# An early Exp-table load, a later second value block, and another step for the next expert's weight split, in a fused attention and mixture-of-experts kernel

## The chip, the core and the metric

The kernel runs on one core of a Trainium2 chip, as one launch. The metric is the device time of the launch in microseconds, as the median of several executions. The host only lays the inputs out.

## What is computed

Sizes: B = H = 8, S = 512, 32 state rows, D = 64; 4352 tokens of 512 channels come out of the attention.

```
scores = x @ state.T / 8 ; xread = softmax(scores) @ state          # every token reads the states
scores2 = state @ x.T / 8 ; sread = softmax(scores2) @ x            # every state reads the tokens
x1 = concat(xread, sread), laid out as [4352, 512]
h  = x1 @ w_in ; x2 = max(0.01*h, h) @ w_out                        # 512 -> 2048 -> 512
e  = argmax(x2 @ w_gate) ; weight = softmax(...)[e] * sigmoid(x2 @ w_output_gate)[e]
out = weight * (relu(x2 @ w1[e]) @ w2[e])                           # 8 experts, 512 -> 1024 -> 512
```

## The kernel before, in words

Every large product is three TensorE (PE) matmuls on numbers split in a high and a low fp32r part (product, L499 to L503: hi times lo, lo times hi, hi times hi). ScalarE (ACT) writes the high parts, VectorE (DVE) subtracts to get the low ones. An order written out by hand sets what each engine does; semaphores join them. There are two phases.

**Phase one** runs over nine blocks b (eight batches and the state rows), each in 16 steps f (layer, L739 on PE, L969 on ACT, L1339 on DVE). The attention's read is folded into the first product: make_v (L528) forms a value block v(b, k), which is the states times 512 columns of w_in; keep_v (ACT, L893) and v_rest (DVE, L1155) split it. Step f does up(b, f) (L618), then down(b, f-2) (L643) into four accumulator banks. Between the two, ACT scales by 0.01 (L927), DVE takes the maximum (L1176), ACT casts to gT_hi (L933), DVE subtracts for gT_lo (L1180). Small work of the neighbouring blocks is put beside these steps (beside_up, L662, and beside_down, L688). For block 0 that is flip_a2 at steps 3 and 4, read_states(0) (L544) at step 4 behind down(0, 2), turn_read(0) (L556) at step 5. The copies that these wait for or feed are DVE's keep_a2 (L1134), keep_read (L1140) and keep_sread (L1145). The eight w_out pieces are split by split_piece (L873, L1074) at the steps that PIECE_AT names.

Before the first step comes a head (L755 to L761): first_scores_T twice, make_v(0, 0), scores_T(0), make_v(0, 1) into acc[0:2]; down(0, 0) writes the same banks, and so waits for v_rest(0, 1) (L648). ACT's head is L1007 to L1015: two exp_rows, keep_v(0, 0), two a_hi, split_piece(0), keep_v(0, 1), two exp_T. DVE's head is L1419 to L1436; its last part is max_T twice, split_piece(0), v_rest(0, 1).

**Phase two** sorts tokens by expert. A step i takes 256 tokens of one expert (tiles = 2), or, as the last step of an expert, 128 (a half step, tiles = 1). Here there are 21 steps for five experts: steps 0 to 10 for the first and largest, 11 to 13, 14, 15 to 17 and 18 to 20; steps 10, 13, 14, 17 and 20 are half steps. Step 0 is written out (L825); steps 1 on are loops. In a step PE does the hidden product (L769, L788) and the output product (L810 to L823), which needs h_lo_done as it goes. DVE's expert_step (L1547) makes hT_lo(0) to hT_lo(4), then turn_quarters(i + 1) (L1329: it transposes the next step's rows xq and copies s_in, once both have landed), then the other three, rows_lo, and the splits. POOL's load_rows (L409) brings the next rows from DRAM: five DMAs on its queue, when s_taken says that the buffer is free.

The next expert's weights are split into w_hi, w_lo (split_expert, L960, L1309; eight pieces, the first four are w1) in the first looped step of an expert (i < first + 1), on ACT behind rows_hi(i + 1), on DVE six behind rows_lo(i + 1) and two at the end of the step. PE starts an expert once e_lo_done tells of its four w1 pieces (L802). SP loads the raw weights (load_planned, L362): w1 when the w1 pieces before are split, w2 when all eight are; the first time behind rows_in 160, the rows of steps 0 and 1. Counts and columns are read from the small tensor ctl, written by DVE (L1500 to L1509). POOL's loop over the experts (L465) reads three of them for each.

Of the kernel before, what the change touches and what calls it, by code (L numbers as in the profile page):

```python
# [26 lines left out]
PIECE_AT = {0: 1, 3: 2, 5: 3, 6: 4, 10: 5, 12: 6, 14: 7}  # L27
# [8 lines left out]
def build(nc, xT_in, x_in, stT_in, st_in, w_in, w_out, w_gates, w1, w2, consts, tri_in, slot_init, out):  # L36
# [7 lines left out]
    with ctx:  # L44
# [238 lines left out]
        CTL_POOL = 35  # L283

# [4 lines left out]
        def _(sp):  # L289
# [70 lines left out]
            sp.wait_ge(rows_in, 160)  # L360
# [22 lines left out]
        def _(pool):  # L383
# [81 lines left out]
            with pool.Fori(0, E) as v:  # L465
                first, end = load_ctl(pool, v + CTL_POOL, MAXP, 1), load_ctl(pool, v + CTL_POOL + 1, MAXP, 1)
                col0 = load_ctl(pool, v + 17, COLS)
                with pool.If(first < end):
                    with pool.Fori(first, end) as sent:
                        n = pool.snap(sent + 2)  # L470
                        col = nc.s_assert_within(pool.snap(col0 + (sent - first) * 2), 0, COLS - 2,
                                                 skip_runtime_bounds_check_because="an expert has room for all tokens")
                        pool.wait_ge(pairs_clear[1], 16 * clear_in(1, PAIRS))
                        pool.wait_ge(s_taken, n)
                        load_rows(col)
                        next_tokens(n)
                        pool.wait_ge(slots_in, 16)
                        pool.wait_ge(toks_shifted, n)
                        pool.tensor_copy(tok_next[:, :], slot_tok[:, bass.ds(col, 2)]).then_inc(toks_kept, 1)
                        scatter(n)  # L480
# [17 lines left out]
        def _(pe):  # L498
# [163 lines left out]
            def beside_up(b, f):  # L662
# [14 lines left out]
                elif f == 5 and r is None:  # L677
# [10 lines left out]
            def beside_down(b, f):  # L688
# [11 lines left out]
                elif f == 4 and r is None:  # L700
# [38 lines left out]
            def layer(b):  # L739

                for f in range(F1):
                    if b == 0 and f == 0:
                        first_up()
                    elif b < B:
                        up(b, f)
                    else:
                        up_states(f)
                    beside_up(b, f)
                    if f >= 2:
                        down(b, f - 2)  # L750
                    beside_down(b, f)
# [7 lines left out]
            pe.wait_ge(half_turned, 2)  # L759
            make_v(0, 1, to=acc[0:2])  # L760
# [111 lines left out]
        def _(act):  # L872
# [39 lines left out]
            def beside_g(b, f):  # L912
                a, r = b + 1 if b < B - 1 else None, b - 1 if b > 0 else None
                if r is not None and f in (1, 2, 4):
# [54 lines left out]
            def layer(b):  # L969
                a, r = b + 1 if b < B - 1 else None, b - 1 if b > 0 else None  # L970
                for f in range(F1):
                    g_step(b, f)
                    if b == 0 and f in PIECE_AT:
# [32 lines left out]

            exp_rows(0, 0)  # L1007
# [5 lines left out]
            keep_v(0, 1, of=acc[0:2])  # L1013
            exp_T(0, 0)
            exp_T(0, 1)  # L1015
# [15 lines left out]
            def expert_step(i, tiles, first, c1, c2, v, s):  # L1031
# [6 lines left out]
                if v + 1 < E:  # L1038
# [21 lines left out]
            c0, c1 = load_ctl(act, 0, MAXP), load_ctl(act, 1, MAXP)  # L1060
            for v in range(E):
                cf = load_ctl(act, v + CTL_FULL, MAXP)
                c2 = load_ctl(act, v + 2, MAXP) if v + 1 < E else c1
                with act.If(c0 < cf):
                    with act.Fori(c0, cf) as i:
                        expert_step(i, 2, c0, c1, c2, v, v % 2)
                with act.If(cf < c1):
                    expert_step(cf, 1, c0, c1, c2, v, v % 2)
                c0, c1 = c1, c2
# [3 lines left out]
        def _(dve):  # L1073
# [362 lines left out]
            v_rest(0, 1, of=acc[0:2])  # L1436
# [53 lines left out]
            def plan_steps():  # L1490
# [15 lines left out]
                dve.tensor_scalar(ctl[:, 26:27], end[:, 7:8], 2.0, None, ALU.add)  # L1506
                dve.tensor_scalar(ctl[:, 44:45], end[:, 7:8], 80.0, 80.0, ALU.mult, ALU.add)
# [39 lines left out]
            def expert_step(i, tiles, first, c1, c2, v, s):  # L1547
# [11 lines left out]
                if v + 1 < E:  # L1559
                    with dve.If(i < first + 1):  # L1560
                        with dve.If(c1 < c2):
                            split_expert(v + 1, 1 - s, range(6))
# [9 lines left out]
                if v + 1 < E:  # L1572
                    with dve.If(i < first + 1):
                        with dve.If(c1 < c2):
                            split_expert(v + 1, 1 - s, range(6, 8))

            c0, c1 = load_ctl(dve, 0, MAXP), load_ctl(dve, 1, MAXP)
            for v in range(E):
                cf = load_ctl(dve, v + CTL_FULL, MAXP)
                c2 = load_ctl(dve, v + 2, MAXP) if v + 1 < E else c1  # L1580
                with dve.If(c0 < cf):
                    with dve.Fori(c0, cf) as i:
                        expert_step(i, 2, c0, c1, c2, v, v % 2)
# [50 lines left out]
```

## Time and profile before

| | us |
|---|---|
| median of 3 runs | 1141.16 (1140.4 to 1143.56) |
| the profiled execution's own time | 1135.01 |
| its span | 1133.3 |
| PE busy in the span | 1106.1 |
| DVE, ACT, POOL busy | 623.1, 401.3, 207.4 |

The span is the profiled execution from its first to its last instruction. PE is busy in 98% of it. Its idle time is the place to look: a wait of PE with an engine named behind it lengthens the kernel by about its own length, since PE has no slack elsewhere.

### The profile page before, as it was taken

How to read it: one execution, taken by the hardware profiler on the slowest of the kernel's cores; microseconds unless marked ns; L12 is line 12 of the kernel's file. 1: busy time of each engine (PE TensorE's matmuls, PEld its weight loads, DVE VectorE, ACT ScalarE, POOL GpSimd, SP SyncE). 2: the span in 40 equal slices, each digit the busy share in tenths (PEclk: the TensorE clock that was granted, in tenths of full speed). 3: DMA queues.
4: the chain of work that ended last, by engine and by line, in shares of the span. 5: the costliest groups of instructions: out<-in, count | busy, mean ns of one | idle time of the engine just before them, and what ended most of it. 6: DMA issues, size and time to landing. Idle time of an engine off the chain costs nothing.

```text
span 1133.3 us, 18114 instructions
## 1 busy us (share of the span) xinstructions
PE 1106.1 (98%) x6514; PEld 895.9 (79%) x6515; DVE 623.1 (55%) x1364; ACT 401.3 (35%) x751; POOL 207.4 (18%) x298
## 2 busy tenths in 40 slices
PE   5999999999999999999999999999999999989997
PEld 2777777777777777777777889989998989878895
DVE  6584484674754854845744566673343336366342
ACT  3444334334434433443344355241121124244121
POOL 1000011020020020110110303532232232333222
PEclk9999999999999999999999999999999999999999
DMA  9398197394692890930130301691111122545111
GB/s 337 115 297 245 57 295 213 123 310 132 186 310 71 247 301 27 307 101 1 38 75 8 124 1 39 149 266 55 56 49 44 37 75 70 168 96 145 40 37 40
DMA packets 73007, 149.85 MB, mean 132 GB/s; under 512 B 11231, under 2 KB 12511, under 8 KB 72928
## 3 DMA queue, kind: packets, MB, share of 16 engines
q1 hardware_dynamic: 59696, 115.34, 35.3%
q0 software_dynamic: 13248, 33.71, 9.8%
q8 instruction: 36, 0.59, 0.2%
q14 instruction: 27, 0.22, 0.1%
HBM read 131.11 MB, written 92.01 MB: 197 GB/s over the span
## 4 chain that ended last, share of the span: by engine, by line
PE 87%; DVE 6%; DMA 3%; ACT 2%; issue 2%; POOLq 0%; POOL 0%; SPq 0%; DVEq 0%; ACTq 0%
PE bank L501 27%; PE bank L503 26%; PE bank L502 26%; PE bank L534 3%; PE bank L552 1%; DMA raw<-w_dram 1%; PE bank L568 1%; DMA s_in<-rows_dram 1%; DVE w_lo L1313 1%; PE bank L576 1%; PE bank L512 1%; ACT w_hi L967 1%; PE bank L541 1%; DVE g_buf L1176 1%; DMA XT<-xT_in_dram 1%
## 5 line engine op out<-in xcount | busy, mean ns | idle before, releaser
L501 PE MATMUL bank<-wout_lo,gT_hi 128*128 128x512 f32 x544 | 215.9, 397 | 0.0
L503 PE MATMUL bank<-wout_hi,gT_hi 128*128 128x512 f32 x544 | 212.3, 390 | 0.0
L502 PE MATMUL bank<-wout_hi,gT_lo 128*128 128x512 f32 x544 | 212.0, 390 | 0.0
L1176 DVE TENSOR_TENSOR g_buf<-g_buf,bank 128x512 f32<-128x512 f32 (+1 forms) x144 | 94.2, 654 | 107.5 <-ACT g_buf L927 107.4
L501 PE MATMUL bank<-xgT_lo,w_hi 128*128 128x256 f32 x512 | 144.8, 283 | 2.9 <-DVE w_lo L1313 2.6
L503 PE MATMUL bank<-xgT_hi,w_hi 128*128 128x256 f32 x512 | 143.8, 281 | 0.0
L502 PE MATMUL bank<-xgT_hi,w_lo 128*128 128x256 f32 x512 | 143.8, 281 | 0.0
L1180 DVE TENSOR_TENSOR gT_lo<-g_buf,gT_hi 128x512 fp32r<-128x512 f32 (+1 forms) x144 | 95.4, 662 | 72.9 <-ACT gT_hi L933 71.4
L927 ACT ACTIVATE g_buf<-bank 128x512 f32<-128x512 f32 (+1 forms) x144 | 82.5, 573 | 147.1 <-PE bank L503 145.6
L933 ACT CAST gT_hi<-g_buf 128x512 fp32r<-128x512 f32 (+1 forms) x144 | 85.9, 597 | 136.5 <-DVE g_buf L1176 136.5
L403 POOL DMA_INDIRECT rows_dram<-y_buf,row_i x34 | 35.0, 1031 | 542.0 <-DVE row_i L1270 534.4
L1022 ACT ACTIVATE hT_hi<-bank 128x256 fp32r<-128x256 f32 x128 | 49.2, 385 | 217.1 <-PE bank L503 217.1
L501 PEld LDWEIGHTS bank<-wout_lo,gT_hi 128*128 128x128 f32 x544 | 102.2, 188 | 26.4 <-DVE gT_lo L1180 5.4
L503 PEld LDWEIGHTS bank<-wout_hi,gT_hi 128*128 128x128 f32 x544 | 102.1, 188 | 22.5
L501 PE MATMUL bank<-w_lo,hT_hi 128*128 128x512 f32 x296 | 116.4, 393 | 2.2 <-DVE hT_lo L1441 1.5
L502 PEld LDWEIGHTS bank<-wout_hi,gT_lo 128*128 128x128 f32 x544 | 102.3, 188 | 20.2
L503 PE MATMUL bank<-w_hi,hT_hi 128*128 128x512 f32 x296 | 115.5, 390 | 0.0
L502 PE MATMUL bank<-w_hi,hT_lo 128*128 128x512 f32 x296 | 115.4, 390 | 0.0
L501 PE MATMUL bank<-aT_lo,v_hi 128*128 128x512 f32 x254 | 107.9, 425 | 2.1 <-DVE g_buf L1176 1.4
L501 PEld LDWEIGHTS bank<-xgT_lo,w_hi 128*128 128x128 f32 x512 | 96.4, 188 | 5.0 <-issue 3.8
L503 PE MATMUL bank<-aT_hi,v_hi 128*128 128x512 f32 x254 | 100.0, 394 | 0.0
L502 PE MATMUL bank<-aT_hi,v_lo 128*128 128x512 f32 x254 | 99.7, 393 | 0.0
(216 smaller groups left out, 1697.3 us busy)
## 6 DMA issues: line engine op xcount, KB each, us to landing
rows_dram<-x_in_dram SPq DMA_DIRECT2D x17, 4128.0 KB, 25.2
xq<-rows_dram POOLq DMA_DIRECT2D x88, 128.0 KB, 2.8
raw<-w_dram SPq DMA_DIRECT2D x20, 512.0 KB, 7.8
raw<-w_dram SPq DMA_DIRECT2D x10, 1024.0 KB, 11.1
X<-x_in_dram SPq DMA_DIRECT2D x8, 1024.0 KB, 12.4
XT<-xT_in_dram SPq DMA_DIRECT2D x7, 1024.0 KB, 5.6
win<-w_in_dram SPq DMA_DIRECT2D x4, 1024.0 KB, 11.9
y_buf<-w_out_dram POOLq DMA_DIRECT2D x6, 512.0 KB, 6.2
```

The costliest lines, as they stand in the source:

```text
L403: pool.indirect_dma_start(out=rows_dram, out_offset=bass.IndirectOffsetOnAxis(ap=row_i[:, t:t + 1], axis=0), in_=y_buf[:, t, :], in_offset ...
L501: pe.matmul(o, l_hi, r_lo, start=first, stop=False)
L502: pe.matmul(o, l_lo, r_hi, start=False, stop=False)
L503: return pe.matmul(o, l_hi, r_hi, start=False, stop=last)
L512: last = pe.matmul(aux[g][NS * c:NS * c + NS, :], stT[a % 2][rows, c, cols], XT[rows, c, :], start=True, stop=True)
L534: last = pe.matmul(to[g][NS * c:NS * c + NS, :], stT[b % 2][rows, c, cols], win[rows, c, VW * k:VW * k + VW], start=True, stop=True)
L541: last = pe.transpose(to[:, P * t:P * t + P], a2T[:, g, P * t:P * t + P], ident)
L927: act.mul(g_buf[:, n, 0:w], up_b[n][:, 0:w], 0.01).then_inc(scaled, 1)
L933: act.copy(gT_hi[f % 4][:, 0:w], g_buf[:, n, 0:w]).then_inc(g_hi_done, 1)
L1022: act.activation(hT_hi[:, f, :], h_b[f % 4][:, :PAIR], ACT.Relu).then_inc(h_hi_done, 1)
L1176: dve.tensor_tensor(g_buf[:, n, 0:w], g_buf[:, n, 0:w], up_b[n][:, 0:w], ALU.max).then_inc(g_ready, 1)
L1180: dve.tensor_tensor(gT_lo[f % 4][:, 0:w], g_buf[:, n, 0:w], gT_hi[f % 4][:, 0:w].bitcast(fp32), ALU.subtract).then_inc(g_lo_done, 1)
```

## The change

For block 0: an Exp on a small tensor is the first thing ACT does; make_v(0, 1) goes behind up(0, 1); keep_v(0, 1) and v_rest(0, 1) go behind the work on step 0; exp_T(0, 1) goes between the two ACT parts of step 0; split_piece(1) goes from step 0 to 1; read_states(0) and turn_read(0) go one step later, and so do keep_read and keep_sread. For the experts: the split of the second expert's weights goes to step 2 (the smallest of 2 and the first expert's last step), the first raw load waits for the rows of step 2 (rows_in 240), and where the step with the split is a half step, the first two pieces go between its parts. POOL's loop over the experts is written out eight times, and the first expert's start is a constant.

```diff
-PIECE_AT = {0: 1, 3: 2, 5: 3, 6: 4, 10: 5, 12: 6, 14: 7}
+PIECE_AT = {1: 1, 3: 2, 5: 3, 6: 4, 10: 5, 12: 6, 14: 7}
...
+        CTL_SPLIT = 45
...
-            sp.wait_ge(rows_in, 160)
+            sp.wait_ge(rows_in, 240)
...
-            with pool.Fori(0, E) as v:
-                first, end = load_ctl(pool, v + CTL_POOL, MAXP, 1), load_ctl(pool, v + CTL_POOL + 1, MAXP, 1)
-                col0 = load_ctl(pool, v + 17, COLS)
...
+            first, col0 = 1, pool.snap(first_col + 4)
+            for v in range(E):
+                end = load_ctl(pool, v + CTL_POOL + 1, MAXP, 1)
+                if v > 0:
+                    col0 = load_ctl(pool, v + 17, COLS)
                 with pool.If(first < end):
                     with pool.Fori(first, end) as sent:
+                        send_step(sent, first, col0)
+                first = end
...
-                elif f == 5 and r is None:
+                elif f == 6 and r is None:
                     turn_read(0)
...
-                elif f == 4 and r is None:
+                elif f == 5 and r is None:
                     read_states(0)
...
+                    if b == 0 and f == 1:
+                        pe.wait_ge(half_turned, 2)
+                        make_v(0, 1, to=acc[0:2])
                     beside_up(b, f)
...
             scores_T(0)
-            pe.wait_ge(half_turned, 2)
-            make_v(0, 1, to=acc[0:2])
...
+                if b == 0 and f == 0:
+                    exp_T(0, 1)
...
                     g_step(b, f)
+                    if b == 0 and f == 0:
+                        keep_v(0, 1, of=acc[0:2])
...
+            act.wait_ge(rank_read, 1)
+            act.activation(edif[:, 0, :], before[:, 0, :], ACT.Exp)
             exp_rows(0, 0)
...
             split_piece(0)
-            keep_v(0, 1, of=acc[0:2])
             exp_T(0, 0)
-            exp_T(0, 1)
...
-            def hidden_rows(i):
+            def hidden_rows(i, piece):
                 for j in range(2):
                     act.wait_ge(h_ready, F2 * i + 4 * j + 1)
                     act.activation(h_rows[:, 4 * P * j:4 * P * j + 4 * P], h_b[j][:, :], ACT.Relu).then_inc(h_hi_done, 1)
+                    if j == 1:
+                        piece(1)
                     act.wait_ge(h_ready, F2 * i + 4 * j + 4)
                     act.copy(hT_hi[:, 4 * j:4 * j + 4, 0:P], h_b[2 + j][:, :].rearrange("p (f t) -> p f t", f=4)).then_inc(h_hi_done, 3)
+                    if j == 0:
+                        piece(0)
...
-                    with act.If(i < first + 1):
-                        with act.If(c1 < c2):
-                            split_expert(v + 1, 1 - s)
+                def pieces(which):
+                    if v + 1 < E:
+                        with act.If(i == split_at):
+                            with act.If(c1 < c2):
+                                split_expert(v + 1, 1 - s, which)
                 if tiles == 2:
                     hidden_T(i)
+                    rows_hi(i + 1)
+                    pieces(range(8))
                 else:
-                    hidden_rows(i)
-                rows_hi(i + 1)
+                    hidden_rows(i, lambda n: pieces((n,)))
+                    rows_hi(i + 1)
+                    pieces(range(2, 8))
...
-            c0, c1 = load_ctl(act, 0, MAXP), load_ctl(act, 1, MAXP)
+            c0, c1, split_at = 1, load_ctl(act, 1, MAXP), load_ctl(act, CTL_SPLIT, 2, 1)
...
-                c0, c1 = c1, c2
+                c0, c1, split_at = c1, c2, c1
...
-                    if b == 0 and f == 1:
+                    if b == 0 and f == 0:
+                        v_rest(0, 1, of=acc[0:2])
+                    elif b == 0 and f == 1:
                         norm_T(0, 0)
                         norm_T(0, 1)
...
                         keep_a2(0, 1, aux[1])
+                    elif b == 0 and f == 5:
                         keep_read(0)
-                    elif b == 0 and f == 5:
+                    elif b == 0 and f == 6:
                         keep_sread(0)
...
             split_piece(0)
-            v_rest(0, 1, of=acc[0:2])
...
+                dve.tensor_scalar(ctl[:, CTL_SPLIT:CTL_SPLIT + 1], end[:, 0:1], -1.0, 2.0, ALU.add, ALU.min)
...
                     h_lo_turned(i, 0)
+                    pieces(range(2))
                     h_lo_turned(i, 1)
                 rows_lo(i + 1)
...
+                pieces(range(2 if tiles == 1 else 0, 6))
...
+                pieces(range(6, 8))
```

## Rows read from the trace of the kernel before

**Rows 1.** The page, part 1: busy time of each engine.
```profile
PE 1106.1 (98%) x6514; PEld 895.9 (79%) x6515; DVE 623.1 (55%) x1364; ACT 401.3 (35%) x751; POOL 207.4 (18%) x298
```

**Rows 2.** Waits of PE: us in total, times, longest us.
```profile
PE bank L501 <- DVE w_lo L1313: 2.6, 1, 2.6
...
PE bank L501 <- DVE hT_lo L1441: 1.8, 2, 1.5
PE bank L609 <- ACT aT_hi L891: 1.7, 1, 1.7
...
PE bank L501 <- DVE g_buf L1176: 1.4, 1, 1.4
```

**Rows 3.** Timeline of PE, head: start, us, instruction, [idle before <-releaser].
```profile
14.19 1.96 PE L534 MATMUL bank<-win,stT 64*32 64x512 f32 x16
...
23.04 0.44 PE L503 MATMUL bank<-aT_hi,v_hi 128*128 128x512 f32 x1
...
26.14 0.39 PE L503 MATMUL bank<-aT_hi,v_hi 128*128 128x512 f32 x1
26.37 0.45 PE L501 MATMUL bank<-wout_lo,gT_hi 128*128 128x512 f32 x1
...
50.08 1.09 PE L534 MATMUL bank<-win,stT 64*32 64x512 f32 x16
```

**Rows 4.** Timeline of ACT and DVE, head.
```profile
10.53 1.28 ACT L887 ACT_TABLE_LOAD   x1 [10.53 <-DVE a_buf L1110]
...
11.83 1.15 ACT L887 ACTIVATE a_buf<-a_buf 128x512 f32<-128x512 f32 x2
...
19.19 1.06 ACT L896 CAST v_hi<-bank 128x512 fp32r<-128x512 f32 x2
...
22.95 1.28 DVE L1158 TENSOR_TENSOR v_lo<-bank,v_hi 128x512 fp32r<-128x512 f32 x2
```

**Rows 5.** Windows: busy us (count) of PE, PEld, DVE, ACT, POOL; PEclk, DMA share, GB/s.
```profile
20.00:22.00 2.00, 2.00 (x5) 1.40 (x5) 1.93 (x7) 1.10 (x4) 0.00 (x0) 0.50 1.06 379
```

**Rows 6.** Timeline of PE, ACT and DVE around read_states(0) and keep_sread(0).
```profile
39.54 1.97 PE L552 MATMUL bank<-X,a_buf 128*64 128x128 f32 x32 [1.10 <-DVE a_buf L1137]
...
43.14 0.60 ACT L927 ACTIVATE g_buf<-bank 128x512 f32<-128x512 f32 x1 [4.97 <-PE bank L503]
...
46.04 0.29 DVE L1149 COPY sread<-bank 64x128 f32<-64x128 f32 x1
```

**Rows 7.** Timeline of SP, POOL, DVE and ACT in steps 1 and 2.
```profile
722.50 1.85 SPq L341 DMA_DIRECT2D raw<-w_dram  x4
...
724.00 2.42 POOL L412 DMA_DIRECT2D xq<-rows_dram  x4 [3.19 <-issue]
...
737.92 1.32 DVE L1332 STREAM_TRANSPOSE bank<-xq 128x512 f32<-128x512 f32 x2 [6.36 <-DMA s_in<-rows_dram]
...
754.93 0.39 ACT L1022 ACTIVATE hT_hi<-bank 128x256 fp32r<-128x256 f32 x1 [1.20 <-PE bank L503]
```

**Rows 8.** Timeline of ACT: the split in step 11, and the start of step 12.
```profile
951.06 7.70 ACT L967 CAST w_hi<-raw 128x1024 fp32r<-128x1024 f32 x8
...
962.18 0.39 ACT L1022 ACTIVATE hT_hi<-bank 128x256 fp32r<-128x256 f32 x1 [3.43 <-PE bank L503]
```

**Rows 9.** Timeline of ACT, DVE and PE in half step 14 and up to step 15.
```profile
998.50 1.32 DVE L1332 STREAM_TRANSPOSE bank<-xq 128x512 f32<-128x512 f32 x2 [2.04 <-issue]
...
1001.91 0.60 ACT L1027 ACTIVATE h_rows<-bank 128x512 f32<-128x512 f32 x1 [0.75 <-PE bank L503]
...
1004.19 0.69 DVE L1446 TENSOR_TENSOR hT_lo<-bank,hT_hi 128x512 fp32r<-128x512 f32 x1 [2.24 <-ACT hT_hi L1029]
...
1005.32 0.39 PE L501 MATMUL bank<-w_lo,hT_hi 128*128 128x512 f32 x1
...
1006.05 6.90 DVE L1313 TENSOR_TENSOR w_lo<-raw,w_hi 128x1024 fp32r<-128x1024 f32 x6
...
1010.82 0.38 PE L501 MATMUL bank<-xgT_lo,w_hi 128*128 128x256 f32 x1 [2.62 <-DVE w_lo L1313]
```

More of the change, by code:

```diff
@@ L463, in _, with send_step @@
             pool.wait_ge(toks_shifted, 2)
-            with pool.Fori(0, E) as v:
-                first, end = load_ctl(pool, v + CTL_POOL, MAXP, 1), load_ctl(pool, v + CTL_POOL + 1, MAXP, 1)
-                col0 = load_ctl(pool, v + 17, COLS)
+            def send_step(sent, first, col0):
+                n = pool.snap(sent + 2)
+                col = nc.s_assert_within(pool.snap(col0 + (sent - first) * 2), 0, COLS - 2,
+                                         skip_runtime_bounds_check_because="an expert has room for all tokens")
+                pool.wait_ge(pairs_clear[1], 16 * clear_in(1, PAIRS))
+                pool.wait_ge(s_taken, n)
+                load_rows(col)
+                next_tokens(n)
+                pool.wait_ge(slots_in, 16)
+                pool.wait_ge(toks_shifted, n)
+                pool.tensor_copy(tok_next[:, :], slot_tok[:, bass.ds(col, 2)]).then_inc(toks_kept, 1)
+                scatter(n)
+            first, col0 = 1, pool.snap(first_col + 4)
[3 more added lines that the diff above has]
+                    col0 = load_ctl(pool, v + 17, COLS)
                 with pool.If(first < end):
                     with pool.Fori(first, end) as sent:
[L470 to L480, printed above, removed]
+                        send_step(sent, first, col0)
+                first = end
             total, after, after2 = load_ctl(pool, 8, MAXP), load_ctl(pool, 25, MAXP + 1), load_ctl(pool, 26, MAXP + 2)
@@ L1065, in _ @@
                     with act.Fori(c0, cf) as i:
-                        expert_step(i, 2, c0, c1, c2, v, v % 2)
+                        expert_step(i, 2, split_at, c1, c2, v, v % 2)
                 with act.If(cf < c1):
-                    expert_step(cf, 1, c0, c1, c2, v, v % 2)
-                c0, c1 = c1, c2
+                    expert_step(cf, 1, split_at, c1, c2, v, v % 2)
+                c0, c1, split_at = c1, c2, c1
         @block.vector
@@ L1544, in _, with expert_step, pieces @@
             dve.tensor_copy(s_now[:, :], s_next[:, :]).then_inc(s_moved, 1)
-            def expert_step(i, tiles, first, c1, c2, v, s):
+            def expert_step(i, tiles, split_at, c1, c2, v, s):
+                def pieces(which):
+                    if v + 1 < E:
+                        with dve.If(i == split_at):
+                            with dve.If(c1 < c2):
+                                split_expert(v + 1, 1 - s, which)
                 if tiles == 2:
@@ L1556, in expert_step @@
                     h_lo_turned(i, 0)
+                    pieces(range(2))
                     h_lo_turned(i, 1)
                 rows_lo(i + 1)
[L1559 to L1562, printed above, removed]
+                pieces(range(2 if tiles == 1 else 0, 6))
                 dve.wait_ge(scattered, 32 * i)
@@ L1571, in expert_step @@
                 dve.tensor_copy(s_now[:, :], s_next[:, :]).then_inc(s_moved, 1)
[L1572 to L1577, printed above, removed]
+                pieces(range(6, 8))
+            c0, c1, split_at = 1, load_ctl(dve, 1, MAXP), load_ctl(dve, CTL_SPLIT, 2, 1)
             for v in range(E):
@@ L1582, in _ @@
                     with dve.Fori(c0, cf) as i:
-                        expert_step(i, 2, c0, c1, c2, v, v % 2)
+                        expert_step(i, 2, split_at, c1, c2, v, v % 2)
                 with dve.If(cf < c1):
-                    expert_step(cf, 1, c0, c1, c2, v, v % 2)
-                c0, c1 = c1, c2
+                    expert_step(cf, 1, split_at, c1, c2, v, v % 2)
+                c0, c1, split_at = c1, c2, c1
 def kernel(x, state, moe_w_in, moe_w_out, moe2_w_gate, moe2_w_output_gate, moe2_w1, moe2_w2):
```

3 lines of the change are left out of this document (1 added, 2 removed).

## The prediction

> **What bounds the kernel now.** I read the page first: PE is busy 1106.1 us of a span of 1133.3 [rows 1], so DVE and ACT matter only where PE waits for them. PE's waits come next. Of those with an engine behind them, five matter here: 2.6 us for w_lo, 1.5 for hT_lo (the longest of two), 1.7 for aT_hi, 1.4 for g_buf and 1.1 for a_buf [rows 2, 6]. The change aims at all five. Each is read in its own stretch of the timeline, to see what would be late next if it went. The most that these waits hold is 8.3 us, or 0.7%.
>
> **The early Exp.** ACT loads its table at 10.53, for 1.28 us, when DVE has already handed over the scores, and the first Exp runs at 11.83 [rows 4]. With the load at the start, where ACT is idle for 10.5 us, that Exp starts 1.3 us earlier, and all that hangs on it (DVE's row sums and transposes, aT_hi, aT_lo, v_lo, up(0, 0)) moves up by 1.3. The added Exp on 8 columns lies in the same idle time and costs nothing.
> The row prices only 1.30 us from load to Exp. The Trainium skill (ScalarE: Activation LUTs, What ACT_TABLE_LOAD costs) adds a drain of about 1380 ns to each switch of table, 2.66 us together; by that rule the head would gain up to 1.4 us more. No such time stands between the two rows of this trace, so I leave it out.
>
> **make_v(0, 1) behind up(0, 1).** Before, it ran from 14.19 in 1.96 us [rows 3], ahead of the wait for aT_hi; now it takes the place of the wait of 1.4 us for g_buf. The work on PE is the same. What decides is the start of down(0, 0), at 26.37 before [rows 3], since behind it PE has much work queued. It needs v_rest(0, 1), and now the chain is make_v, ACT, DVE:
> - up(0, 1) ended at 23.04 + 0.44 = 23.5 [rows 3]; less 1.3 it is 22.2.
> - make_v(0, 1) takes 1.96 us where the clock is low and 1.09 in the steady state [rows 3]. The granted clock is 0.50 from 20 to 22 us [rows 5], that is 1.2 GHz of 2.4, after a stretch in which PE had waited 1.7 us. The last matmul of up(0, 1) is already shorter. I take the low clock for two thirds of make_v: it ends at 22.2 + 1.6 = 23.8. The ends are 23.3 (all at full clock) and 24.2 (all low).
> - ACT copies two halves in 1.06 us and DVE subtracts two in 1.28 [rows 4], one half behind the other: 23.8 + 0.5 + 1.3 = 25.6.
> So down(0, 0) starts 0.8 us earlier (between 0.3 and 1.3). PE waits 0.5 us for it, since up(0, 2) needs only g of step 0. DVE is free for that at 22.95 - 1.3 = 21.7 [rows 4], as v_rest now stands behind it, and an operation of that size takes 0.7 (as the 0.69 of [rows 9]): 22.4, before make_v ends. ACT's keep_v now stands ahead of its scaling for step 1, which ends near 25.4; that g follows at 26.3 and up(0, 3), at about 28.3, does not wait. split_piece(1) at step 1 delays only g of step 2, which up(0, 4) wants at some 33 us.
>
> **read_states(0) one step later.** It waited 1.10 us at 39.54 for DVE's keep_a2 [rows 6]. Behind up(0, 5) and down(0, 3) its input is 3 us old: +1.1. What is late next is keep_sread(0), which make_v(0, 2) needs in the same step now. From ACT's scaling at 43.14 to the end of the second copy at 46.04 + 0.29 it is 3.2 us [rows 6]; PE has turn_read and a down (0.3, and 12 matmuls of 0.23, the distance from 26.14 to 26.37 [rows 3]) = 3.05, and some latency is to be added: a new wait of 0.3 (bounds 0 and 1.2, the latter where DVE is still at split_piece(3)). Net +0.8. Head in all: 0.8 + 0.8 = 1.6, between 0 and 2.4.
>
> **Second expert's split, and its loads.** Before, SP issues the weights at 722.50, POOL the rows of step 2 at 724.00, behind them; the rows are there at 737.92, where DVE had sat idle for 6.36 us [rows 7], with hT_lo(5) queued behind that transpose. Hence PE's 1.5. Now SP waits for those rows, which have the DMA engines to themselves: the wait goes, +1.5. In step 2, PE is also 0.16 us late behind the split at the end of step 1 (ACT's 1.20 where its neighbours have 1.04) [rows 7]: +0.15. What it costs: the same eight pieces go to step 2, a full step in the middle of an expert. The split in full step 11 shows what that does: ACT is done in 7.70 us and then idle for 3.43 until the next step's first hidden block [rows 8], and no wait of PE follows. So nothing; if that cover were gone, each us of ACT would be one of PE. Of the moved queues: SP has only later experts' loads behind its wait, and step 11 is 180 us away. POOL's rows for step 3 are now issued near 734 and compete with 4 MB of weights; before, rows in that place came 13.9 us after their first issue (724.00 to 737.92). That gives 748, while DVE asks for them near 754: nothing. POOL loads fewer registers ahead of 724.00, so its 3.19 us of issue before that can only shrink; one more DVE operation on one number is under 0.2 us and no wait of PE stands there. Sum: +1.65.
>
> **Half step 14.** This is the costly one: expert 2 has one half step, and its split must be ready when it ends. DVE starts six pieces at 1006.05, 1.15 us each, and the fourth is done as PE restarts at 1010.82 after 2.62 us [rows 9]. Now DVE does two pieces between the parts of hT_lo. ACT's two copies of 0.96 (7.70 / 8 [rows 8]) fall into its idle time of 0.75 ahead of 1001.91 and the one after it [rows 9]. Piece 0 runs from 1001.1 to 1002.1, the Relu behind it to 1002.7, piece 1 to 1003.7; DVE's part of piece 1 (1.2) is done at 1004.95, and hT_lo's second half at 1005.6 rather than at 1004.88; PE wants it at 1005.32 [rows 9]: a new wait of 0.3. rows_lo then ends at 1006.75, two pieces at 1009.05, and PE, due at 1008.2 + 0.3, waits 0.6. So 2.62 becomes 0.9: +1.7, of which I keep 1.5 for the added branches. Bounds 0.5 and 2.0.
>
> **Sum.** 1.6 + 1.65 + 1.5 = 4.75 us. The profiled execution, 1135.01, would become 1130.3. The median is 6.15 us above that execution; I carry that offset over: 1141.16 - 4.75 = 1136.4. A measurement here can tell about 0.3%, or 3.4 us, from no change.
>
> **Rivals.**
> 1. The head gives nothing: PE works little between 14.5 and 17.1 us now, and the clock stays low through make_v (+0.4) and up(0, 2), six matmuls at twice their distance of 0.23 us, less what one waits anyway (+1.2). For: the clock is at 0.50 right behind a wait today [rows 5]. Against: PE has one wait less between 17 and 24 us. Gain 4.75 - 1.6 = 3.15: 1138.0. Chance 0.15. The Trainium skill (TensorE: Matmul & The Clock Gate, Part 1) says that the throttled state is the default and activity releases it; by that rule the idle stretch works against this change, and its price is this rival's.
> 2. DVE's two early pieces hold up hT_lo, and the half step gives nothing: PE would wait 1.6 us longer at the fifth output block than my 0.3. For: the cover is 0.44 us only (1004.88 to 1005.32). Against: the pieces are counted from rows. Gain 3.25: 1137.9. Chance 0.12.
> 3. The load of the table is not moved by the early Exp, as it is placed by the compiler. Then down(0, 0) starts no earlier: gain 3.95, 1137.2. Chance 0.06.
> 4. Slower: in all five half steps ACT and DVE now pass three conditional parts more than one. If each branch cost them long issue time, ACT's Relu and cast would be late. Cover: 0.75 us ahead of 1001.91 plus 0.3 until PE needs it, and 2.24 on DVE [rows 9]. The longest issue wait of DVE here is 2.04, at a change of expert with its register loads [rows 9]. At 2.7 us a branch each half step would lose 1.6, or 8.2 in all, which undoes the gain and makes the kernel 3.4 slower: 1144.6. Below 1.05 us a branch nothing is lost. Chance 0.05.
> 5. More than forecast, 1135.0: full clock at the head and the drain saved. Chance 0.07.
>
> **Numbers.** Forecast 1136.4, chance 0.55, own range 1134.5 to 1137.7. The range must take in rivals 1 to 3 and the runs' own spread of 3 us: 1133 to 1140. Faster by over 0.3%: 0.55 + 0.07 + 0.04 of rival 3 = 0.66; within: 0.15 + 0.12 + 0.02 = 0.29; slower 0.05.
>
> **What would show it.** Right: the table load near 1 us and the first Exp near 10.5; down(0, 0) near 25.6; a wait of about 0.5 on v_lo; read_states without one; about 0.3 on sread ahead of make_v(0, 2); no hT_lo wait near 739; in half step 14 waits of 0.3 and 0.6. Wrong: a clock of 0.50 beyond 24 us; rows of step 3 that land after 754; a wait over 1 us at the half step's fifth output block; new waits in steps 10, 13, 17 and 20, which would speak for rival 4.

## The result, and the profile after

| | before | after |
|---|---|---|
| median, five runs each | 1141.16 (1139.18 to 1143.56) | 1133.39 (1132.32 to 1134.07) |
| the profiled execution's own time | 1135.01 | 1132.32 |
| its span | 1133.3 | 1130.6 |

The ratio is 0.9933, with an interval of 0.992 to 0.9945: 7.8 us faster, or 0.7%, clearly past the 0.3% that can be told from no change. The time lies inside the wide range (1133 to 1140), near its lower end, and below the prediction's own narrower one (1134.5 to 1137.7); the forecast gain was 4.75. One thing does not fit: the medians are 7.8 us apart and the two profiled spans only 2.7. The profiled execution of before, 1135.01, is not one of the five and lies 4.2 below the lowest of them. The experiments had to explain both that gap and the 3 us beyond the forecast.

The page of the kernel after, part 1, answers to [rows 1]: PE works about as long as before (1.3 us more), so that what this pair of profiles gains is idle time.

```profile
PE 1107.4 (98%) x6514; PEld 895.5 (79%) x6515; DVE 624.0 (55%) x1365; ACT 401.5 (36%) x752; POOL 206.9 (18%) x297
```

PE's waits in the same profile (line waited for: total, times, longest) answer to [rows 2]:

```profile
PE bank L616 <- ACT aT_hi L899: 1.9, 2, 1.7
...
PE bank L566 <- DVE scT L1163: 0.9, 5, 0.2
PE bank L508 <- DVE gT_lo L1200: 0.9, 1, 0.9
...
PE bank L508 <- DVE v_lo L1178: 0.6, 2, 0.5
PE bank L508 <- DVE w_lo L1333: 0.5, 1, 0.5
PE bank L541 <- DVE sread L1169: 0.3, 1, 0.3
```

Of the five waits that the change aimed at, those for hT_lo, a_buf and g_buf are gone, w_lo has shrunk from 2.6 to 0.5, and the 1.7 for aT_hi stays (it now comes 1.3 earlier). The new ones for v_lo (0.5) and sread (0.3) were forecast. Those for scT and gT_lo were not, and come back below. The timeline of the kernel after, at the places of [rows 3, 4, 7, 9]:

```profile
0.86 1.28 ACT L1020 ACT_TABLE_LOAD   x1 [0.86 <-PEq L1652]
...
7.49 1.11 PE L532 MATMUL bank<-XT,stT 64*32 64x256 f32 x16 [1.31 <-DMA XT<-xT_in_dram]
10.35 0.63 ACT L895 ACTIVATE a_buf<-a_buf 128x512 f32<-128x512 f32 x1 [7.99 <-DVE a_buf L1130]
...
22.11 1.11 PE L541 MATMUL bank<-win,stT 64*32 64x512 f32 x16
...
25.31 0.50 PE L508 MATMUL bank<-wout_lo,gT_hi 128*128 128x512 f32 x1 [0.49 <-DVE v_lo L1178]
...
48.32 1.09 PE L541 MATMUL bank<-win,stT 64*32 64x512 f32 x16 [0.31 <-DVE sread L1169]
...
724.46 2.42 POOL L413 DMA_DIRECT2D xq<-rows_dram  x4 [1.89 <-DVE s_next L1357]
...
733.23 1.85 SPq L342 DMA_DIRECT2D raw<-w_dram  x4
733.23 1.31 DVE L1352 STREAM_TRANSPOSE bank<-xq 128x512 f32<-128x512 f32 x2
...
1001.89 1.23 DVE L1333 TENSOR_TENSOR w_lo<-raw,w_hi 128x1024 fp32r<-128x1024 f32 x1 [0.18 <-ACT w_hi L977]
1003.32 1.23 DVE L1333 TENSOR_TENSOR w_lo<-raw,w_hi 128x1024 fp32r<-128x1024 f32 x1 [0.20 <-ACT w_hi L977]
1004.47 0.68 DVE L1468 TENSOR_TENSOR hT_lo<-bank,hT_hi 128x512 fp32r<-128x512 f32 x1
...
1008.75 0.38 PE L508 MATMUL bank<-xgT_lo,w_hi 128*128 128x256 f32 x1 [0.52 <-DVE w_lo L1333]
```

The reader sees every step of the change where the diff puts it: the table load on an idle ACT, make_v(0, 1) at 22.11, SP's loads at 733.23, and two w_lo pieces ahead of the last hT_lo of the half step. DVE's transposes start at 733.23 as well, with no idle time before them, but neither starts as the rows land. The last of the rows, s_in, is issued at 726.9 and lands 3.4 us later, at 730.3; the transposes stand behind hT_lo(4) on DVE, and SP, which waited until 730.3, issues 2.9 later (load_planned reads three numbers of ctl in between). In the kernel before, the same load took 11.5 us, beside the weights. From the views of the line that issues s_in, first before (L414), then after (L415):

```profile
DMA to landing us min/median/max: 11.5/11.5/11.5
```

```profile
DMA to landing us min/median/max: 3.4/3.4/3.4
```

### The profile page after: what moved, and what is told of

Its sections match the earlier page's. It is cut to its first block, busy times and chain, and to the rows that moved or that the text cites. A ratio compares the mean times of both kernels' runs of the same rounds, so it can differ in the third digit from the quotient of the medians.

```text
span 1130.6 us, 18025 instructions
## 1 busy us (share of the span) xinstructions
PE 1107.4 (98%) x6514; PEld 895.5 (79%) x6515; DVE 624.0 (55%) x1365; ACT 401.5 (36%) x752; POOL 206.9 (18%) x297
## 4 chain that ended last, share of the span: by engine, by line
PE 90%; DVE 5%; DMA 2%; issue 1%; ACT 1%; POOL 0%; DVEq 0%; SPq 0%; ACTq 0%; POOLq 0%
PE bank L508 28%; PE bank L510 27%; PE bank L509 26%; PE bank L541 3%; PE bank L559 2%; DMA raw<-w_dram 1%; PE bank L575 1%; DVE w_lo L1333 1%; PE bank L583 1%; PE bank L519 1%; PE bank L548 1%; DMA XT<-xT_in_dram 0%; DVE g_buf L1196 0%; PE bank L793 0%; DVE gT_lo L1200 0%
## 5 line engine op out<-in xcount | busy, mean ns | idle before, releaser
L1463 DVE SCALAR_TENSOR_TENSOR hT_lo<-bank,hT_hi 128x256 fp32r<-128x256 f32 x128 | 53.4, 424 | 87.4 <-ACT hT_hi L1034 83.7
```

The lines of the kernel that those rows point to most:

```text
L1463: dve.scalar_tensor_tensor(hT_lo[:, f, :], h_b[f % 4][:, :PAIR], 0.0, hT_hi[:, f, :].bitcast(fp32), ALU.max, ALU.subtract).then_inc(h_lo_d ...
```

## The experiments

The theory was that three independent parts (head, second expert, half step 14) give about 1.6, 1.65 and 1.5 us, and that the first profile of after holds something of its own. Its rivals: the parts work on each other, one part gives most of the 7.8, or the profile of before was a mild execution. exp_only, vmove_only, read_only and pool_only were timed once, the others in several rounds. Line numbers shift by a few between kernels. "Ratio" is the time over that of the kernel before on the same chip, whose median was 1141.16, 1137.68, 1136.52 and 1137.18 in the four sessions, so that plain times of different sessions are not compared.

### Both kernels once more

before_again is the kernel before, unchanged.

> The kernel before, unchanged, to see a second profiled execution. Known: its median is 1141.16 us, but its profiled execution took 1135.01; the kernel after has a median of 1133.39 and a profiled execution of 1132.32. Theory A (the row loads of step 2 race with 4 MB of weights, and the first profile showed a mild case): the second profile has PE's wait for hT_lo near 740 us longer than 1.5 us, up to 8, and the rest of the timeline as in the first. Theory B (the product blocks run at a slightly different pace in different executions: in the kernel after each of the blocks 1 to 6 was 0.37 us longer than in the first profile of before, around turn_read, and 1.07 us went ahead of the last down of the state block): the second profile has those losses too, 2.2 and 1.1 us, and hT_lo's wait stays at 1.5. Against the kernel before the ratio is 1.000 by both, within 0.002.

Measured: ratio 1.0 (0.999 to 1.001). Its profile is not that of the first one, though: the span is 1136.0, 2.7 us more than 1133.3. PE's waits:

```profile
PE bank L501 <- DVE w_lo L1313: 2.6, 1, 2.6
PE bank L501 <- DVE hT_lo L1441: 2.5, 2, 1.3
...
PE bank L501 <- DVE xgT_lo L1326: 0.3, 1, 0.3
```

and in its timeline, behind the same wait for hT_lo as in [rows 2], a second wait for hT_lo, and ACT waiting for raw weights:

```profile
740.55 0.50 PE L501 MATMUL bank<-w_lo,hT_hi 128*128 128x512 f32 x1 [1.35 <-DVE hT_lo L1441]
...
747.31 3.89 ACT L967 CAST w_hi<-raw 128x1024 fp32r<-128x1024 f32 x4 [2.96 <-DMA raw<-w_dram]
...
755.11 0.38 PE L501 MATMUL bank<-xgT_lo,w_hi 128*128 128x256 f32 x1 [1.11 <-DVE hT_lo L1441]
...
1012.67 0.38 PE L501 MATMUL bank<-xgT_lo,w_hi 128*128 128x256 f32 x1 [2.59 <-DVE w_lo L1313]
```

In step 1 the first four pieces (w1) are split at once; the other four wait for w2 to land. Here it landed late, DVE's last pieces ran until 754.7, and step 2's hT_lo stood behind them. So the race between rows and weights costs PE 1.35 here, then 1.11, where the first profile shows the one wait of 1.50 alone. The third difference is the clock behind the wait of half step 14. Windows of before_again (us, busy and count of PE, PEld, DVE, ACT, POOL; granted clock; DMA share; GB/s):

```profile
1013.00:1016.00 3.00, 3.00 (x17) 3.00 (x16) 2.90 (x5) 1.88 (x3) 0.37 (x2) 0.53 0.63 173
1016.00:1018.00 2.00, 2.00 (x17) 2.00 (x16) 2.00 (x2) 0.39 (x1) 1.78 (x2) 0.85 1.03 205
```

and of the first profile of before, in the same place behind its wait:

```profile
1012.00:1016.00 4.00, 4.00 (x36) 4.00 (x35) 3.90 (x5) 1.70 (x4) 2.01 (x3) 1.00 1.00 225
```

PE is busy all the time in both, but does 17 matmuls in 3 us in one and 36 in 4 in the other: at a granted clock of 0.53 on average, that is mostly at 1.2 GHz of 2.4, against 1.00. Set matmul by matmul against the first profile, before_again loses 1.3 us there and gets 0.6 of it back by 1042: the three profiles with the long wait and a full clock behind it wait 0.30 to 0.54 for hT_lo in step 16, the seven with a low clock do not. The low clock costs 0.7 to 0.8 in the end.

Of the two theories neither came: the wait near 740 did not grow, a second one came behind it, and the pace of the blocks is that of the first profile within 0.1.

after_again is the kernel after, once more.

> The kernel after, unchanged, for a second profiled execution. In the first, PE waited 0.2 us at turn_read in each of blocks 1 to 6 with another 0.2 lost beside it (0.37 a block, 2.2 in all), and 0.93 us for gT_lo at 698 us; the semaphore of read_states reached DVE and SP 1.3 us after its last matmul. If that belongs to the execution or its chip, this profile has neither, and is some 3 us shorter in span for the same head and expert part. If it belongs to the new program (its longer POOL or ACT code), both are there again. The median should be 0.993 to 0.994 of before either way.

Measured: ratio 0.9937 (0.992 to 0.9953), span 1127.0, 3.6 less than after's first profile. PE's waits, all but one of 0.2 that no engine ended:

```profile
PE bank L532 <- DMA stT<-stT_in_dram: 5.1, 1, 5.1
PE bank L616 <- ACT aT_hi L899: 2.0, 2, 1.7
PE bank L541 <- DMA win<-w_in_dram: 1.9, 1, 1.9
PE bank L532 <- DMA XT<-xT_in_dram: 1.3, 1, 1.3
PE bank L508 <- DVE wch_lo L1337: 0.7, 2, 0.5
PE bank L508 <- DVE v_lo L1178: 0.6, 2, 0.5
PE bank L508 <- DVE w_lo L1333: 0.5, 1, 0.5
PE bank L541 <- DVE sread L1169: 0.3, 1, 0.3
```

The waits for scT and gT_lo are absent, so the change does not bring them (more of this under the offset, below). before_again to after_again is 1136.0 - 1127.0 = 9.0 us. Set matmul by matmul, PE gains 2.24 in the head, 3.46 at the second expert and 3.19 at half step 14, and loses 0.35 later: 8.5, the rest lying outside those matmuls. Each part is sized below from its own kernel too.

### The head: exp_only, vmove_only, read_only, head_only

exp_only has the early Exp alone:

```diff
+            act.wait_ge(rank_read, 1)
+            act.activation(edif[:, 0, :], before[:, 0, :], ACT.Exp)
```

vmove_only moves make_v(0, 1) behind up(0, 1) with its copies, exp_T(0, 1) and split_piece(1); read_only moves read_states, turn_read, keep_read and keep_sread one step; head_only does all three.

> Only the early Exp. Everything from the first Exp to gT_lo(0) hangs on one chain, so down(0, 0) should start 1.3 us earlier than in the kernel before, near 25.1 (26.37 and 26.7 in its two profiles), as early as with the moved make_v(0, 1) (25.2 to 25.6). If so the move of the value block bought nothing by itself. Rival (the moved block does its own share): down(0, 0) at 25.8 or later here.

> Only make_v(0, 1), its splits, exp_T(0, 1) and split_piece(1) moved, without the early Exp. My chain gives down(0, 0) at 23.8 + 1.3 for make_v's end and 1.8 for ACT and DVE: 26.5 to 26.9, so no gain over before (0 within 0.3 us at PE's 150th matmul). Rival: it gains 0.7 or more by itself.

> Only read_states(0) and turn_read(0) one step later. The wait of 1.0 to 1.1 us before read_states(0) goes and one of 0.3 us for sread comes: 0.75 us earlier from PE's 300th matmul on.

> Only the parts of the change in block 0: early Exp, make_v(0, 1) and its splits later, read_states(0) and turn_read(0) one step later. The comparison of the two profiles gives 1.67 us at index 300 of PE's matmuls, so this kernel should be 1.7 us faster than before (ratio 0.9985) by both theories. If the median gain of the whole change (7.8 us) sat in the head for some reason that the profiles do not show, it would be 5 us or more (0.9955).

head_only: ratio 0.9986 (0.9976 to 0.9997), or 1.6 us. The single times of the others can't tell so little, but the trace can. One thing has to be taken out first: the second first_scores_T starts when XT has landed, anywhere from 7.5 to 9.1 us by the execution. From the timeline, first exp_only, then before (the seventh matmul of down(0, 0)), then vmove_only:

```profile
7.57 1.11 PE L525 MATMUL bank<-XT,stT 64*32 64x256 f32 x16 [1.22 <-DMA XT<-xT_in_dram]
...
23.48 0.50 PE L501 MATMUL bank<-aT_lo,v_hi 128*128 128x512 f32 x1 [2.66 <-DVE g_buf L1178]
...
25.34 0.63 PE L501 MATMUL bank<-wout_lo,gT_hi 128*128 128x512 f32 x1
...
27.89 0.43 PE L501 MATMUL bank<-wout_lo,gT_hi 128*128 128x512 f32 x1
```

```profile
27.81 0.40 PE L501 MATMUL bank<-wout_lo,gT_hi 128*128 128x512 f32 x1
```

```profile
8.23 1.11 PE L525 MATMUL bank<-XT,stT 64*32 64x256 f32 x16 [1.73 <-DMA XT<-xT_in_dram]
...
27.04 0.50 PE L501 MATMUL bank<-wout_lo,gT_hi 128*128 128x512 f32 x1 [0.48 <-DVE v_lo L1161]
```

| kernel | XT's matmuls | down(0, 0) | between them | XT to down's 7th matmul | XT to make_v(0, 2) |
|---|---|---|---|---|---|
| before | 7.70 | 26.37 | 18.67 | 20.11 | 42.38 |
| before_again | 8.02 | 26.69 | 18.67 | 20.12 | 42.40 |
| exp_only | 7.57 | 25.34 | 17.77 | 20.32 | 41.76 |
| vmove_only | 8.23 | 27.04 | 18.81 | 20.30 | 42.28 |
| read_only | 9.05 | 27.71 | 18.66 | 20.09 | 41.61 |
| head_only | 8.30 | 25.58 | 17.28 | 18.77 | 40.24 |
| after | 7.49 | 25.31 | 17.82 | 19.33 | 40.83 |
| after_again | 7.51 | 25.17 | 17.66 | 19.15 | 40.62 |
| early_make_v (below) | 8.85 | 25.43 | 16.58 | 18.05 | 39.52 |

At the start of down(0, 0) the early Exp alone gives 0.9, and the later make_v nothing: -0.14 by itself, between -0.05 and 0.5 with the Exp. It trades the wait for g_buf against one for v_lo. But that is too early a place to count. In exp_only, up(0, 2) starts 1.27 earlier (15.91 behind XT's matmuls against 17.18), after a wait for g_buf of 2.66 where before has 1.40, and then the granted clock falls. A window of exp_only (where before has 1.00 in every window from 25 us on):

```profile
25.00:26.00 1.00, 1.00 (x4) 0.81 (x3) 0.94 (x1) 0.52 (x2) 0.00 (x0) 0.50 1.05 387
```

The first six matmuls of down(0, 0) come 0.43 apart instead of 0.23, and at the seventh the gain is gone (20.32 against 20.11). By make_v(0, 2) 0.6 of it is back, as the wait for a_buf at read_states(0) has shrunk from 1.10 to 0.21. The kernels with make_v(0, 1) in that place keep a full clock at down(0, 0); those with the Exp as well are 1.0 to 1.5 ahead of exp_only at the seventh matmul, and gain 1.6 to 2.1 up to make_v(0, 2). So the two edits belong together in these traces. (The seventh matmul lies ahead of read_states(0), so the third edit has no part in that comparison; in the 1.6 to 2.1 it has.) How often the clock falls with the Exp alone, one execution cannot say. It falls with the old head too: pool_only, step2_only and sp240_only, whose head is that of before, have 19.0 to 19.9 to down(0, 0) and 42.9 to 43.1 to make_v(0, 2), where half_only and step2_sp160 have the 18.7 and 42.4 of before.

read_only shows no wait at read_states and the new one of 0.31 for sread; 1.10 - 0.31 is the forecast 0.8, and the table has 0.8.

### The second expert: step2_only, sp240_only, step2_sp160, pool_only

step2_only has both halves of this part, the split in step 2 (on ACT and DVE) and the later loads; sp240_only has the loads alone, step2_sp160 the split alone:

```diff
+                dve.tensor_scalar(ctl[:, CTL_SPLIT:CTL_SPLIT + 1], end[:, 0:1], -1.0, 2.0, ALU.add, ALU.min)
...
-                    with act.If(i < first + 1):
+                    with act.If(i == split_at):
...
-            sp.wait_ge(rows_in, 160)
+            sp.wait_ge(rows_in, 240)
```

> Only the split of the second expert's weights in step 2, and its first raw load behind the rows of step 2 (rows_in 240). By the first profile it is worth 1.65 us (ratio 0.9985). Theory A: 4 to 6 us (0.995 to 0.9965), as the race with the weights is gone in every execution, and the spread of its times falls from 4 us to 2. Theory B: 1.65 us, and the spread stays.

> Only the wait of the first raw load for the rows of step 2; the split stays in step 1. The wait for hT_lo near 740 goes (+1.4 to 2), but ACT's split in step 1 now starts with weights issued near 733, some 10 us later: its w2 pieces end near 752 rather than 749, and the first hidden blocks of step 2 wait for ACT, 3 us. Net: 1 to 2 us slower than before (ratio 1.001 to 1.002). Rival: as much time is won as lost, 1.000.

> Only the split moved to step 2; the raw loads still go ahead of the rows of step 2. The wait for hT_lo near 740 stays (1.4 to 2 us), the one at the start of step 2 (0.16 us in the first profile, 1.11 in the second) goes. Gain 0.2 to 1.1 us (ratio 0.999 to 1.000). Together with the wait of SP alone this shows whether the 3.45 us of both need both. Rival (the clock falls in some executions behind a longer wait, and that is where the rest of the 3.45 came from): more than 1.5 us here as well.

| kernel | ratio | us |
|---|---|---|
| step2_only | 0.9973 (0.9962 to 0.9983) | -3.1 |
| sp240_only | 1.0078 (1.0062 to 1.0095) | +8.9 |
| step2_sp160 | 1.0001 (0.999 to 1.0012) | 0 |

The part gives 3.1 (1.9 to 4.3 by its interval), more than the forecast 1.65, and neither half gives anything alone. In step2_only there is no wait for hT_lo at either place. In the eight profiles with the old order of split and loads these waits come to 1.26 to 2.46, 1.84 in the mean. Set between the same two matmuls (the 3950th and the 4400th), the first profile of before is 0.5 faster than the mean of the eight, and the four profiles with the whole part are 1.4 to 1.8 faster than that first profile: about 2.2 us are seen in the traces, and whether the rest of the 3.1 is more than the error of the measurement is not shown.

The spread of the times points to the race as what changes from execution to execution. By theory A it was to fall from 4 us to 2 and the gain to be 4 to 6, by theory B neither. In the same session eight executions of step2_only lie within 0.9 us, twelve each of before_again, head_only and half_only within 2.9, 4.9 and 2.5. In all sessions the kernels whose weights wait for the rows of step 2 stay within 0.9 to 1.8 (4 to 8 executions each), the others within 2.5 to 4.9 (5 to 31). So the spread falls as in theory A, and the gain lies between the two.

The split alone was to give 0.2 to 1.1 and gives 0 (1.4 lost to 1.1 gained). It keeps the wait for hT_lo (1.48 in its trace), since the weights still run against the rows. The loads alone were expected to cost 1 to 2 us and cost 9. Timeline of sp240_only:

```profile
732.97 1.85 SPq L341 DMA_DIRECT2D raw<-w_dram  x4
...
747.13 3.90 ACT L967 CAST w_hi<-raw 128x1024 fp32r<-128x1024 f32 x4 [10.19 <-DMA raw<-w_dram]
...
760.27 0.58 PE L501 MATMUL bank<-xgT_lo,w_hi 128*128 128x256 f32 x1 [8.14 <-DVE hT_lo L1441]
```

```profile
760.00:764.00 4.00, 3.73 (x20) 3.73 (x21) 1.56 (x6) 0.38 (x1) 2.06 (x2) 0.60 1.04 202
```

In the timeline ACT's first four pieces start at 747.13, after 10.19 idle, where before had them at 739.76, with the second four and the next step's Relu queued behind them; PE waits 8.14 for hT_lo, and then works at a granted clock of 0.60 (windows, second fence). Expecting 1 to 2, I had counted how late the weights are, and not that ACT does nothing in the meantime.

pool_only is the edit of POOL's loop alone: eight copies of the body, the first start a constant.

> Only POOL's loop over the experts written out. My theory of the sum gives it no time of its own: 1.000. If the written-out code is what delays turn_read in blocks 1 to 6, its profile shows waits of 0.2 us for scT there and the blocks are 0.37 us longer. The rows of step 2 are issued up to 2 us earlier (after 722 rather than 724) if POOL's register loads were what held them.

A single time, 1135.93, gives no verdict. In its timeline the rows of step 2 go out with 1.94 of idle time before them, ended by DVE's s_next, where [rows 7] has 3.19 of issue:

```profile
723.39 2.42 POOL L412 DMA_DIRECT2D xq<-rows_dram  x4 [1.94 <-DVE s_next L1343]
```

There is then no wait at 740, but one of 1.26 for hT_lo at 753.80: the race falls otherwise. No wait for scT shows, which speaks against POOL's loop as what put it into after's first profile; after_again, which has the same loop and no such wait, speaks against it too.

### The half step: half_only

The two pieces between the parts of a half step, with the split left in the first looped step (on DVE the same way):

```diff
+                def pieces(which):
+                    if v + 1 < E:
+                        with act.If(i < first + 1):
+                            with act.If(c1 < c2):
+                                split_expert(v + 1, 1 - s, which)
...
-                    hidden_rows(i)
-                rows_hi(i + 1)
...
+                    hidden_rows(i, lambda n: pieces((n,)))
+                    rows_hi(i + 1)
+                    pieces(range(2, 8))
```

> Only the first two pieces of a split put between the parts of a half step. In the profiles PE's wait at the start of step 15 went from 2.62 to 0.52 us. Both theories: 1.9 to 2.1 us faster (ratio 0.998), new waits in half step 14 under 0.5 us together. The rival that branches cost issue time in all five half steps: no gain, or slower.

Measured: ratio 0.9979 (0.9971 to 0.9988), 2.4 us against 1.5 in the prediction and 1.9 to 2.1 in the expectation. Its timeline, and the windows behind the wait:

```profile
1009.82 0.38 PE L501 MATMUL bank<-xgT_lo,w_hi 128*128 128x256 f32 x1 [0.52 <-DVE w_lo L1321]
```

```profile
1012.00:1016.00 4.00, 4.00 (x35) 3.90 (x35) 3.90 (x7) 0.98 (x3) 2.84 (x4) 1.00 1.03 217
```

The wait is 0.52 and the clock stays at 1.00. Over all profiles: ten show the long wait (2.6), and in seven of them the clock then falls (not in before, step2_only and vmove_only); four show the short one (after, after_again, half_only, early_make_v), and in none of them does it fall. The part saves 2.1 us of that wait. It pays 0.25 for it at the fifth output block, where two matmuls come 0.33 behind their forerunner instead of 0.23; the first of them in the kernel after, 0.34 behind the one at 1004.87:

```profile
1005.21 0.50 PE L508 MATMUL bank<-w_lo,hT_hi 128*128 128x512 f32 x1
```

So 1.82 us are saved when PE starts step 15, the same in all four profiles, and where the clock would have fallen 0.7 to 0.8 more. At seven in ten that makes 2.3 to 2.4, near the measured gain.

The three parts together: 0.9986 x 0.9973 x 0.9979 = 0.9938, against 0.9933 and 0.9937 measured. They add up within their intervals, which are some 1 us to either side for each.

### A version with make_v back in its place: early_make_v

The starts of down(0, 0) in the head's table suggest taking the early Exp without the later make_v. In early_make_v the changed kernel has make_v(0, 1) and keep_v(0, 1) back where before has them, and v_rest(0, 1) within DVE's work on step 0:

```diff
-                    if b == 0 and f == 1:
-                        pe.wait_ge(half_turned, 2)
-                        make_v(0, 1, to=acc[0:2])
...
+            pe.wait_ge(half_turned, 2)
+            make_v(0, 1, to=acc[0:2])
...
+                if b == 0 and f == 0:
+                    v_rest(0, 1, of=acc[0:2])
```

> The kernel after, but make_v(0, 1) back in PE's wait for aT_hi and its ACT copy in ACT's idle time ahead of exp_T(0, 0); DVE's subtraction stays behind the maximum of step 0 (now between that and gT_lo(0)), so g of step 0 is not held up. Then up(0, 2) starts near 22.2 instead of 23.0, and down(0, 0) near 24.2 instead of 25.2. 1.0 us faster than the kernel after: ratio to before 0.9928 where the kernel after has 0.9933 and 0.9937. Rival (the second w_in chunk lands late, as in three profiles where make_v(0, 1) waited 0.5 to 1.0 us for it, and delays aT_hi's product): no gain over the kernel after.

```profile
8.85 1.11 PE L532 MATMUL bank<-XT,stT 64*32 64x256 f32 x16 [2.57 <-DMA XT<-xT_in_dram]
...
25.43 0.47 PE L508 MATMUL bank<-wout_lo,gT_hi 128*128 128x512 f32 x1 [0.23 <-DVE gT_lo L1200]
```

From XT's matmuls to down(0, 0) it is 16.58, some 1.1 less than in after and after_again, and 39.52 to make_v(0, 2), 1.1 to 1.3 less. Its wait for g_buf is 1.48 and the clock stays full. Against exp_only, whose make_v(0, 1) stands in the same place, what is moved is v_rest(0, 1), exp_T(0, 1) and split_piece(1): with these copies in their new places (v_rest no longer stands ahead of DVE's maximum of step 0) the gain comes without the move of make_v. No run moves v_rest alone. The time does not prove it: ratio 0.9927 (0.9913 to 0.994), whose interval holds the 0.9933 and 0.9937 of the changed kernel. XT landed 1.3 later in this execution, so its span, 1127.8, is no shorter than after_again's. The trace says that it is the better head by about 1 us; the times leave it open.

## Why the prediction was right or wrong

- **Direction and wide range: right; the size short by 3.** Each of the three parts is faster by its own interval. The time is inside the wide range and below the own one (1134.5 to 1137.7): two terms of the sum were too small, and so was what was read into the offset.
- **The early Exp: right.** The load at 0.86, the first Exp at 10.35 against 11.83, of which 0.2 is XT's luck, so 1.3. In exp_only up(0, 2) starts 1.27 earlier; at down(0, 0) it is 0.9, as the clock has fallen behind the wait for g_buf.
- **The drain that the Trainium skill adds** (ScalarE: Activation LUTs, What ACT_TABLE_LOAD costs): the trace shows 1.3 and not 2.66, so nothing of it for this first load on an idle engine; no run here shows a switch from one table to another.
- **make_v(0, 1): right by the sum, and not by its terms.** Down(0, 0) at 25.31 against 25.6, with 0.49 of wait against 0.5. But make_v ran at full clock (1.11) from 22.11, where I had 1.6 for a mostly low one. The sum went by the start of down(0, 0) and gave no price to each edit: vmove_only costs 0.14 there, and exp_only gains 0.9 there and loses it to a low clock within six matmuls. What the pair buys is the Exp's 1.3 with a clock that stays full; the prediction had the low clock as a danger of the changed kernel, and these runs show it in exp_only and in three kernels with the old head.
- **read_states: right**, 0.31 of new wait against 0.3.
- **The second expert: mechanism right, mis-sized, 1.65 against 3.1.** That the split could move for nothing held: no wait of PE behind step 2 in after. The mis-sized term is the one behind "Hence PE's 1.5": it took the cost of a race from one execution. In before_again the same race costs 1.35 at once and 1.11 a step later; in pool_only 1.26 in the other place only; over eight profiles 1.84 in the mean. Moved out of the race, all of that goes. The traces account for about 2.2 of the 3.1; the interval (1.9 to 4.3) leaves open whether more is missing.
- **Half step 14: mechanism right, mis-sized, 1.5 against 2.4.** The two waits that I expected in its place came as 0.25 at the fifth output block (0.3 forecast) and 0.52 (0.6): 1.82 was saved, where the sum had 1.7, and no branch cost shows that 0.2 had to be kept for. The rest is the clock, 0.7 to 0.8 us net in seven of ten profiles, of which the first profile of before had none. I had looked for a low clock at the head alone.
- **The offset: wrong.** "I carry that offset over" held the 6.15 us between the profiled execution and the median to be the same for both kernels. It was 1.07 for the kernel after. Two things were in it. One is what the change removes: the second wait for hT_lo and the low clock, which the profiled execution of before happened not to have; before_again's span is 2.7 longer. The other is the level of the first session. The five times of before there (1139.18 to 1143.56) lie above every one of its 65 later times (1134.82 to 1139.16), and the profiled execution, 1135.01, lies among the later ones. The five of after (1132.32 to 1134.07) lie in the same way above the four of after_again (1128.52 to 1129.71). So both kernels took some 3.5 to 4.6 us more in the first session, with the same ratio, and only after was profiled at that level. Its scT and gT_lo waits come with 3.3 us between the 300th and the 3900th matmul, most of that difference. Less these 2.7 and 3.6, the 9.0 between the second profiles are the 2.7 between the first.
- **Rivals.** 1: the clock was full at make_v in all four profiles that have it there. 2: 0.25 at the fifth output block instead of 1.6 more. 3: the load moved. 4: steps 10, 13, 17 and 20 show no new wait in after and after_again; half_only has one of 0.54 for hT_lo at 1062.00, in step 17; early_make_v's 0.49 at 1034.30, in step 16, is where before waits 0.32 too. 5 came nearest in size: its full clock came, its drain did not, and the rest has other reasons than it names.

**Open.** In the first profile of after PE waits about 0.2 for scT in blocks 1 to 6, and each block is 0.37 longer, 2.2 in all. The timeline shows this for one block:

```profile
160.91 1.97 PE L559 MATMUL bank<-X,a_buf 128*64 128x128 f32 x32
...
164.20 0.42 DVE L1163 COPY scT<-bank 128x256 f32<-128x256 f32 x1 [2.21 <-PE bank L559]
```

PE's last matmul of that group ends near 162.9, and the copy behind it starts 1.3 later. No other profile has it, after_again's included, and no other profile has the level of the first session. As all five times of after there are at least 2.6 above after_again's, it was probably in each of them; whether the kernel before had it there no profile shows, and its cause was not found.

## What to carry to other kernels

A race between small row loads and a large weight load has no single cost: take two or three profiles of the kernel before, and price the race by their mean, and expect the spread of the times to fall with it. Where two edits aim at one chain, cost each without the other, and count at a place far enough behind: here one seemed to give the whole gain at the start of down(0, 0), and had lost it six matmuls later. Before an offset is carried from a profile to a median, see that both are of one session. A move of the consumer and the later load that feeds it belong together: the load alone cost 9 us, the consumer alone gave nothing, both gave 3.

## What the hardware showed that was not expected

- After a wait of 2.6 us in which PE did nothing, the granted clock fell (0.53 over the next 3 us in before_again) in seven profiles of ten, at the same instructions; the price was 1.3 us, of which 0.6 came back where PE would have waited later. After a wait of 0.5 there it fell in none of four.
- Two profiles of one kernel differed by 2.7 us (before) and 3.6 us (after) in some 1130, and the landing of one load alone moves by 1.6 (XT, 7.5 to 9.1 us).
- Raw loads issued 10 us later (732.97 against 722.50) made the kernel 8.9 us slower, by one engine that stood at its wait with the next step's work behind it.
- Five row loads issued ahead of the weights instead of behind them landed 3.4 us after the last issue instead of 11.5.
